# Giving a query with an empty bucket all keys alike, in a bucketed attention kernel

## The chip, the cores and the metric

One core of one Trainium2 chip runs the whole program in one launch. The metric is device time in microseconds from start to end of an execution; the median of several runs is given. TensorE (PE) multiplies matrices, VectorE (DVE) reduces and combines, ScalarE (ACT) does exponentials and copies, GpSimd (POOL) does elementwise work in SBUF, SyncE (SP) issues the DMAs.

## The reference

Attention with hashed buckets over 2 batches, 8 heads, 768 positions of 64 values, and behind it two feed-forward stages. Only the attention is touched:

```python
q_bits = (np.einsum('bhsd,dk->bhsk', q, proj) > 0)      # six bits a query
k_bits = (np.einsum('bhsd,dk->bhsk', k, proj) > 0)
mask = q_bucket[..., :, None] == k_bucket[..., None, :]
scores = scale * np.matmul(q, k.transpose(0, 1, 3, 2))
scores = np.where(mask, scores, -1000000000.0)
scores = scores - np.max(scores, axis=-1, keepdims=True)
attn = np.exp(scores)
attn = attn / (np.sum(attn, axis=-1, keepdims=True) + 1e-09)
out = np.matmul(attn, v)
```

A query whose bucket holds no key ("lone") has -1e9 in its whole row; after the subtraction of the maximum every entry is 0, so it takes all 768 keys with equal weight. The stages behind are max(x w1, x w2, x w3) w_out on 1536 tokens, and a gated one with 2048 hidden columns.

## The kernel before, in words

The order of each engine's work is written out by hand, one function for each engine, and semaphores order the engines among each other. The attention has 96 tiles, each of 128 queries against 768 keys. They are taken in 32 groups of three; n is the group, p = n // 4 the pair of heads and st = n % 4 the stage in the pair.

For tile i: TensorE (`scores`, L1027) multiplies the queries by the keys twice, the second time (76 rows) adding 2^100 for each bit that differs, so the mask is part of the product, with its sign turned. VectorE (`row_max`, L790) takes the minimum of the negated scores into one column of `neg_max`. ScalarE (`exp_tile`, L624) writes `probs[i % 6]` and adds up the row into `sums`. VectorE (`invert_sums`, L795) adds 1e-9 and takes the reciprocal, and GpSimd (`norm`, L468) multiplies the tile by it. TensorE (`turn_probs`, L1047) transposes the tile in two halves into one of three banks of a ring (`psR`), ScalarE and VectorE copy these to `probs_t` (L637, L810), and TensorE (`times_values`, L1054) multiplies by the values.

What waits for what around the change: `scores(i)` waits for the exponential of tile i - 2 (L1031), since there are two score banks. `turn_probs` waits for the norm of its tile and for a free bank. Within group n VectorE's order is row_max(3n), copy_turned, invert_sums(3n-1, 1) (one tile), row_max(3n+1), invert_sums(3n, 2) (two tiles), in stage 2 make_bits, in even groups x_lo_unit, row_max(3n+2), copy_turned (L845 to L863). GpSimd's order is norm(3n-1), norm(3n), norm(3n+1), then in stages 0 and 1 make_qk_hi and make_qk_lo (L447 to L458) for the next pair, in stage 2 mark (L460), and in stages 2 and 3 of pairs 4 to 6 three steps of sums_of_x (L506), in the last pair first_block (L531 to L548). ScalarE also copies the turned q and k of the next pair (L621), and TensorE needs the same ring banks for them. SyncE moves the split q and k and the marks to their places by DMA once GpSimd has made them (L340 to L360), and loads ahead.

For a lone query of the kernel before, the exponentials are those of the keys with the fewest differing bits, since each differing bit adds 2^100 and the minimum is subtracted.

The program's second part, the two feed-forward stages, follows from about 232 us on and is not edited. GpSimd splits the weights there (L445, L490, L579), VectorE has instructions with two SBUF inputs there (`h_lo`, L937, for one).

Of the kernel before, what the change touches and what calls it, by code (L numbers as in the profile page):

```python
# [5 lines left out]
def lsh_attention_ffn(nc, q, k, v, proj, w1, w2, w3, w_out, w_in2, w_out2, out):  # L6
    F32, F32R, BF16 = mybir.dt.float32, mybir.dt.float32r, mybir.dt.bfloat16
    I32 = mybir.dt.int32
    ALU, ACT, AX = mybir.AluOpType, mybir.ActivationFunctionType, mybir.AxisListType
    ts = bass.ts  # L10

    B, H, S, D = q.shape
# [3 lines left out]
    P = 128  # L16
# [8 lines left out]
    UPS2 = F2 // P  # L25
    NEG_SCALE = -1.0 / 8.0
    assert D == 64 and H * D == DM and NBITS == 6
    MASKED = 2.0 ** 100
    CONSTS = 2
    WARM_UP = 22  # L30

# [3 lines left out]
    PROBS = 6  # L35
# [44 lines left out]
    with ctx:  # L80
        def sb(name, shape, dt):
            return ctx.enter_context(nc.sbuf_tensor(name, shape, dt))

        def sem(name):
            return ctx.enter_context(nc.semaphore(name))
# [12 lines left out]
        neg_max = sb("neg_max", [P, 6], F32)  # L98
        sums = sb("sums", [P, 6], F32)
        guarded = sb("guarded", [P, 6], F32)  # L100
        inv = sb("inv", [P, 6], F32)
        with ExitStack() as attention:
            probs = [attention.enter_context(nc.sbuf_tensor(f"probs{i}", [P, S], F32)) for i in range(PROBS)]

# [105 lines left out]
        scores_ready = sem("scores_ready")  # L210
        max_ready = sem("max_ready")
        probs_ready = sem("probs_ready")
        sums_guarded = sem("sums_guarded")
        inv_ready = sem("inv_ready")
        probs_normed = sem("probs_normed")
# [218 lines left out]
        def _(pool):  # L434
# [32 lines left out]

            def norm(i):  # L468
                pool.wait_ge(inv_ready, 2 * (i // 3) + (2 if i % 3 == 2 else 1))
                pool.tensor_scalar(probs[i % PROBS][:, :], probs[i % PROBS][:, :], inv[:, i % 6:i % 6 + 1], 1.0,  # L470
                                   ALU.mult, ALU.mult).then_inc(probs_normed, 1)

            def raw_part(k, name):

# [56 lines left out]
            for n in range(GROUPS + 1):  # L531
                p, st = n // 4, n % 4
                if n > 0:
                    norm(3 * n - 1)
                if n < GROUPS:
                    norm(3 * n)
                    norm(3 * n + 1)
                    if st == 2 and p + 1 < PAIRS:
                        mark(p + 1)
                    if st < 2 and p + 1 < PAIRS:  # L540
                        make_qk_hi(2 * p + 2 + st)
                        make_qk_lo(2 * p + 2 + st)
                    if PAIRS // 2 <= p < PAIRS - 1 and st >= 2:
                        for step in range(6 * (p - PAIRS // 2) + 3 * st - 6, 6 * (p - PAIRS // 2) + 3 * st - 3):
                            if step < 16:
                                sums_of_x(step)
                    if p == PAIRS - 1:
                        first_block(st)  # L548
# [232 lines left out]
        def _(dve):  # L781
# [13 lines left out]
            def invert_sums(i, count):  # L795
                cols = slice(i % 6, i % 6 + count)
                turn = 2 * (i // 3) + (1 if i % 3 == 2 else 0)
                dve.wait_ge(probs_ready, i + count)
                dve.tensor_scalar(guarded[:, cols], sums[:, cols], 1e-9, None, ALU.add).then_inc(sums_guarded, 1)
                dve.wait_ge(sums_guarded, turn + 1)  # L800
                if i >= 6:
                    dve.wait_ge(probs_normed, i - 6 + count)
                dve.reciprocal(inv[:, cols], guarded[:, cols]).then_inc(inv_ready, 1)  # L803

            def copy_turned(i, j):
# [20 lines left out]
            dve.tensor_scalar(marks[:, 3:4], row[:, :], float(3 * NBITS), None, ALU.is_ge).then_inc(marks_made, 1)  # L826
            dve.tensor_scalar(marks[:, 1:2], row[:, :], float(MARKS), MASKED, ALU.is_ge, ALU.mult).then_inc(marks_made, 1)
            dve.wait_ge(marks_made, 3)
# [16 lines left out]
            for n in range(GROUPS + 1):  # L845
                p, st = n // 4, n % 4
                if n < GROUPS:
                    row_max(3 * n)
                if n > 0:
                    copy_turned(3 * n - 3, 0)  # L850
                    invert_sums(3 * n - 1, 1)
                if n < GROUPS:
                    row_max(3 * n + 1)
                if n < GROUPS:
                    invert_sums(3 * n, 2)
                    if st == 2 and p + 1 < PAIRS:
                        make_bits(("bits", p + 1), slice(0, P))
                if n >= 4 and n % 2 == 0:
                    x_lo_unit(n // 2 - 2)
                if n < GROUPS:  # L860
                    row_max(3 * n + 2)
                if n > 0:
                    copy_turned(3 * n - 1, 1)  # L863
# [383 lines left out]
```

## Time and profile before

| what | value |
|---|---|
| median of 3 runs | 693.0 us (692.21 to 694.57) |
| the profiled execution's own time | 692.77 us |
| its span (first to last instruction) | 690.3 us |
| PE busy | 679.4 us, 98% |
| DVE busy | 378.3 us, 55%, 683 instructions |
| ACT busy | 274.7 us, 40% |
| POOL busy | 395.0 us, 57% |
| granted TensorE clock | full throughout |

The shares are over the whole span. A busy VectorE or GpSimd costs time only where TensorE, or the last chain of waits, stands behind it. So each row below is read with its place in time: the loop over groups lasts from about 14 to 232 us.

### The profile page before, as it was taken

Reading aid. Unit: us, or ns where it says so; the run is one execution under the profiler, and the core shown is the slowest. Engines: PE = TensorE matmul, PEld = TensorE weight load, DVE = VectorE, ACT = ScalarE, POOL = GpSimd, SP = SyncE. Lnnn points to the kernel's source line nnn. Section 1 sums busy time; section 2 is a strip of 40 time slices with the busy share of each in tenths; the row PEclk is TensorE's granted clock in tenths of the full one; section 3 lists DMA queues with packets and bytes.
Section 4 is the critical chain, followed back from the end, with each engine's and each line's share of the span. In section 5 each row is a group of like instructions: output and inputs, shape, how many; then the busy total and the mean of one; then the engine's idle time right before and its main releaser. Section 6 shows DMA issues by size and latency. Waiting matters only on the chain.

```text
span 690.3 us, 11104 instructions
## 1 busy us (share of the span) xinstructions
PE 679.4 (98%) x3970; PEld 592.9 (86%) x3970; DVE 378.3 (55%) x683; ACT 274.7 (40%) x582; POOL 395.0 (57%) x448
## 2 busy tenths in 40 slices
PE   7899999999999999999999999999999999999998
PEld 5677777777777699999999999999999999999996
DVE  5767676767677799879688613222222242222222
ACT  3877787877777530110105113222222232222222
POOL 4755755688876899778843123444444444444441
PEclk9999999999999999999999999999999999999999
DMA  5845736628342111101010111222222152222202
GB/s 116 201 108 131 174 85 148 162 81 185 97 110 85 32 31 30 31 32 54 24 46 1 62 31 46 62 62 62 61 62 62 46 168 65 71 64 64 71 20 91
DMA packets 67141, 54.07 MB, mean 78 GB/s; under 512 B 29200, under 2 KB 56080, under 8 KB 67088
## 3 DMA queue, kind: packets, MB, share of 16 engines
q1 hardware_dynamic: 66768, 53.36, 29.1%
q8 instruction: 32, 0.52, 0.3%
q14 instruction: 21, 0.17, 0.1%
q10 hardware_dynamic: 320, 0.01, 0.0%
HBM read 32.51 MB, written 3.15 MB: 52 GB/s over the span
## 4 chain that ended last, share of the span: by engine, by line
PE 91%; DVE 5%; DMA 1%; SPq 1%; issue 1%; ACT 0%; DVEq 0%; ACTq 0%
PE psS L1043 10%; PE psO L1065 9%; PE psR L1051 9%; PE psR L1113 8%; PE psR L1111 8%; PE psR L1112 8%; PE psS L1111 5%; PE psS L1113 5%; PE psS L1112 5%; PE psS L1213 4%; PE psS L1214 4%; PE psS L1212 4%; DVE probs L869 2%; PE psR L1012 2%; PE psO L1214 1%; PE psO L1213 1%
## 5 line engine op out<-in xcount | busy, mean ns | idle before, releaser
L445 POOL TENSOR_SCALAR w_hi<-w_raw 128x512 fp32r<-128x512 f32 (+2 forms) x134 | 84.1, 629 | 199.8 <-PE psO L1214 129.7
L979 DVE TENSOR_TENSOR probs_t<-psR,probs_t 128x384 f32<-128x384 f32 x64 | 35.7, 557 | 181.9 <-ACT probs_t L761 181.9
L470 POOL TENSOR_SCALAR probs<-probs,inv 128x768 f32<-128x768 f32 x96 | 86.1, 905 | 66.4 <-DVE inv L803 65.3
L761 ACT ACTIVATE probs_t<-psR 128x384 f32<-128x384 f32 x64 | 31.5, 492 | 188.0 <-PE psR L1113 188.0
L792 DVE TENSOR_REDUCE neg_max<-psS 128x1 f32<-128x768 f32 x96 | 91.7, 956 | 20.3 <-PE psS L1043 15.9
L579 POOL TENSOR_TENSOR w_lo<-w_raw,w_hi 128x512 fp32r<-128x512 f32 (+1 forms) x68 | 90.6, 1332 | 5.7
L628 ACT ACTIVATE probs<-psS,neg_max 128x768 f32<-128x768 f32 x96 | 86.4, 900 | 11.8 <-DVE neg_max L792 11.8
L1051 PE MATMUL psR<-ident,probs 128*128 128x128 f32 x576 | 74.6, 273 | 1.5 <-ACT w_raw L621 0.9
L637 ACT ACTIVATE probs_t<-psR 128x384 f32<-128x384 f32 x128 | 59.4, 491 | 34.2 <-PE psR L1051 34.1
L1051 PEld LDWEIGHTS psR<-ident,probs 128*128 128x128 f32 x576 | 66.5, 141 | 6.0 <-POOL probs L470 1.9
L1065 PE MATMUL psO<-probs_t,v_raw 128*64 128x384 f32 x384 | 68.8, 494 | 0.0
L1111 PE MATMUL psR<-x_hi,w_hi 128*128 128x384 f32 x176 | 59.1, 336 | 0.0
L1113 PE MATMUL psR<-x_hi,w_lo 128*128 128x384 f32 x176 | 59.0, 335 | 0.0
L1112 PE MATMUL psR<-x_lo,w_hi 128*128 128x384 f32 x176 | 58.9, 335 | 0.0
L1065 PEld LDWEIGHTS psO<-probs_t,v_raw 128*64 128x64 f32 x384 | 24.8, 136 | 30.9 <-issue 30.7
L1214 PE MATMUL psS<-w_hi,stacks 128*128 128x512 f32 x128 | 50.4, 394 | 0.0
L1213 PE MATMUL psS<-w_lo,stacks 128*128 128x512 f32 x128 | 50.4, 393 | 0.0
L1212 PE MATMUL psS<-w_hi,stacks 128*128 128x512 f32 x128 | 49.8, 389 | 0.0
L490 POOL TENSOR_TENSOR w_lo<-w_raw,w_hi 128x256 fp32r<-128x256 f32 x52 | 45.2, 876 | 0.3
L982 DVE TENSOR_TENSOR stacks<-probs_t,stacks 128x384 fp32r<-128x384 f32 x64 | 37.5, 587 | 3.8
L1113 PE MATMUL psR<-h_hi,w_lo 128*128 128x384 f32 x116 | 39.0, 336 | 0.0
L1111 PE MATMUL psR<-h_hi,w_hi 128*128 128x384 f32 x116 | 38.9, 336 | 0.0
(204 smaller groups left out, 1533.8 us busy)
## 6 DMA issues: line engine op xcount, KB each, us to landing
w_raw<-in_moe_w_in SPq DMA_DIRECT2D x32, 256.0 KB, 2.6
w_raw<-in_moe_w_out SPq DMA_DIRECT2D x32, 256.0 KB, 2.7
w_raw<-in_moe_w SPq DMA_DIRECT2D x9, 512.0 KB, 3.8
h_lo<-w_hi SPq DMA_DIRECT2D x22, 192.0 KB, 3.6
h_hi<-w_hi SPq DMA_DIRECT2D x18, 192.0 KB, 3.7
w_raw<-in_q SPq DMA_DIRECT2D x16, 192.0 KB, 3.3
w_raw<-in_k SPq DMA_DIRECT2D x16, 192.0 KB, 4.1
v_raw<-in_v SPq DMA_DIRECT2D x16, 192.0 KB, 2.6
```

The lines of the kernel that those rows point to most:

```text
L445: return pool.tensor_scalar(dst, src, 1.0, 1.0, ALU.mult, ALU.mult)
L470: pool.tensor_scalar(probs[i % PROBS][:, :], probs[i % PROBS][:, :], inv[:, i % 6:i % 6 + 1], 1.0, ALU.mult, ALU.mult).then_inc(probs_norm ...
L579: pool.tensor_tensor(w_lo[:, cols], src, f32(w_hi[:, cols]), ALU.subtract).then_inc(done, 1)
L628: act.activation(probs[i % PROBS][:, :].rearrange("p (a b) -> p a b", a=2), psS[i % 2][:, :, 0:HALF], ACT.Exp, bias=neg_max[:, i % 6:i % 6 ...
L792: dve.tensor_reduce(neg_max[:, i % 6:i % 6 + 1], psS[i % 2][:, :, 0:HALF], AX.XY, ALU.min).then_inc(max_ready, 1)
L1051: mm = pe.transpose(o[:, ts(c, P)], probs[i % PROBS][:, ts(j * TH + c, P)], ident[:, :])
L1065: mm = pe.matmul(psO[a * D:(a + 1) * D, 0:HALF], v_raw[p % 2][a][:, c, :], probs_t[u % 2][:, a, c, :], start=c == 0, stop=c == NT - 1)
L1111: pe.matmul(o, wh, xh, start=c == 0, stop=False)
L1112: pe.matmul(o, wh, xl, start=False, stop=False)
L1113: mm = pe.matmul(o, wl, xh, start=False, stop=c == len(terms) - 1)
L1213: pe.matmul(acc[t], g_part(g % 2, 0)[:, ts(t, P)], wl, start=False, stop=False)
L1214: mm = pe.matmul(acc[t], g_part(g % 2, 1)[:, ts(t, P)], wh, start=False, stop=f == UPS2 - 1)
```

## The change

`invert_sums` first derives two values from the row maximum: `lone` is 2^60 where the minimum of the negated scores is at least 2^99 (no key in the bucket) and 0 elsewhere, `lone_sums` is 768 times that. The sum's addition of 1e-9 also adds `lone_sums`, now a tensor in SBUF, and `norm` adds `lone` to each entry before it multiplies by the reciprocal. The wait for the norms of six tiles ago moves from before the reciprocal to the front of the function.

```diff
+    LONE = 2.0 ** 60
...
+        lone = sb("lone", [P, 6], F32)
+        lone_sums = sb("lone_sums", [P, 6], F32)
...
             def norm(i):
                 pool.wait_ge(inv_ready, 2 * (i // 3) + (2 if i % 3 == 2 else 1))
-                pool.tensor_scalar(probs[i % PROBS][:, :], probs[i % PROBS][:, :], inv[:, i % 6:i % 6 + 1], 1.0,
-                                   ALU.mult, ALU.mult).then_inc(probs_normed, 1)
+                pool.tensor_scalar(probs[i % PROBS][:, :], probs[i % PROBS][:, :], lone[:, i % 6:i % 6 + 1],
+                                   inv[:, i % 6:i % 6 + 1], ALU.add, ALU.mult).then_inc(probs_normed, 1)
...
             def invert_sums(i, count):
                 cols = slice(i % 6, i % 6 + count)
                 turn = 2 * (i // 3) + (1 if i % 3 == 2 else 0)
-                dve.wait_ge(probs_ready, i + count)
-                dve.tensor_scalar(guarded[:, cols], sums[:, cols], 1e-9, None, ALU.add).then_inc(sums_guarded, 1)
-                dve.wait_ge(sums_guarded, turn + 1)
                 if i >= 6:
                     dve.wait_ge(probs_normed, i - 6 + count)
+                dve.wait_ge(max_ready, i + count)
+                dve.tensor_scalar(lone[:, cols], neg_max[:, cols], MASKED / 2, LONE, ALU.is_ge, ALU.mult).then_inc(lone_found, 1)
+                dve.tensor_scalar(lone_sums[:, cols], neg_max[:, cols], MASKED / 2, S * LONE, ALU.is_ge,
+                                  ALU.mult).then_inc(lone_found, 1)
+                dve.wait_ge(probs_ready, i + count)
+                dve.wait_ge(lone_found, 2 * turn + 2)
+                dve.scalar_tensor_tensor(guarded[:, cols], sums[:, cols], 1e-9, lone_sums[:, cols], ALU.add,
+                                         ALU.add).then_inc(sums_guarded, 1)
+                dve.wait_ge(sums_guarded, turn + 1)
                 dve.reciprocal(inv[:, cols], guarded[:, cols]).then_inc(inv_ready, 1)
```

## Rows read from the trace of the kernel before

**Rows 1.** Busy time by stretch: busy us (instructions) of each engine, clock, DMA share.

```profile
70.00:97.50 27.50, 27.50 (x192) 20.25 (x188) 19.27 (x39) 21.16 (x47) 16.58 (x17) 1.00 0.59 136
```

**Rows 2.** Waits from 30 to 232 us: total us, times, longest.

```profile
DVE guarded L799 <- ACT probs L628: 31.8, 30, 1.1
...
DVE neg_max L792 <- PE psS L1043: 15.1, 22, 1.2
```

**Rows 3.** Timeline, stage 0's end and stage 1: start, duration us, instruction, [idle before].

```profile
153.30 1.05 ACT L621 ACTIVATE w_raw<-psR,qk_scale 128x384 f32<-128x384 f32 x2
...
154.12 1.15 PE L1051 MATMUL psR<-ident,probs 128*128 128x128 f32 x9
...
155.81 1.15 PE L1051 MATMUL psR<-ident,probs 128*128 128x128 f32 x9
...
157.35 0.14 DVE L799 TENSOR_SCALAR guarded<-sums 128x1 f32<-128x1 f32 x1
157.53 0.16 DVE L803 RECIPROCAL inv<-guarded 128x1 f32<-128x1 f32 x1
...
157.69 0.96 DVE L792 TENSOR_REDUCE neg_max<-psS 128x1 f32<-128x768 f32 x1
...
159.71 0.17 DVE L799 TENSOR_SCALAR guarded<-sums 128x2 f32<-128x2 f32 x1 [1.06 <-ACT probs L628]
...
161.99 0.42 PE L1043 MATMUL psS<-h_lo 128*128 128x384 f32 x1
```

**Rows 4.** Timeline at the start: two independent 128x1 instructions of VectorE.

```profile
2.23 0.14 DVE L826 TENSOR_SCALAR marks<-row 128x1 f32<-128x1 int32 x1
2.29 0.14 DVE L827 TENSOR_SCALAR marks<-row 128x1 f32<-128x1 int32 x1
```

**Rows 5.** Timelines: VectorE's instructions that fell on running ones of GpSimd.

```profile
24.06 0.90 POOL L470 TENSOR_SCALAR probs<-probs,inv 128x768 f32<-128x768 f32 x1
...
24.73 0.26 DVE L799 TENSOR_SCALAR guarded<-sums 128x2 f32<-128x2 f32 x1 [1.06 <-ACT probs L628]
...
377.38 2.02 POOL L579 TENSOR_TENSOR w_lo<-w_raw,w_hi 128x768 fp32r<-128x768 f32 x1
...
377.62 2.20 DVE L937 TENSOR_TENSOR h_lo<-probs_t,h_lo 128x384 fp32r<-128x384 f32 x1
```

**Rows 6.** GpSimd: the norm's form (busy us, mean ns), then two instructions of the timeline.

```profile
L470 POOL TENSOR_SCALAR probs<-probs,inv 128x768 f32<-128x768 f32 x96 | 86.1, 905 | 66.4 <-DVE inv L803 65.3
...
154.97 0.83 POOL L445 TENSOR_SCALAR w_hi<-w_raw 128x768 fp32r<-128x768 f32 x1
...
155.89 1.82 POOL L458 TENSOR_TENSOR w_lo<-w_raw,w_hi 128x768 fp32r<-128x768 f32 x1
```

**Rows 7.** Timeline of a stage 2 group, after one addition of a stage 3.

```profile
150.79 1.00 POOL L519 TENSOR_TENSOR early<-early 128x384 f32<-128x384 f32 x1
...
162.85 1.82 POOL L458 TENSOR_TENSOR w_lo<-w_raw,w_hi 128x768 fp32r<-128x768 f32 x1
...
164.31 0.14 DVE L799 TENSOR_SCALAR guarded<-sums 128x1 f32<-128x1 f32 x1
...
167.55 0.62 DVE L787 TENSOR_SCALAR bits<-psR,marks 128x384 f32<-128x384 f32 x1 [0.51 <-PE psR L1023]
...
168.55 0.94 DVE L792 TENSOR_REDUCE neg_max<-psS 128x1 f32<-128x768 f32 x1
...
169.53 0.91 ACT L628 ACTIVATE probs<-psS,neg_max 128x768 f32<-128x768 f32 x1
...
170.81 0.94 PE L1043 MATMUL psS<-stacks 128*128 128x384 f32 x4
```

**Rows 8.** The chain of waits at the start: start us, us, what.

```profile
28.73 0.97 DVE neg_max L792
...
31.78 0.52 PE psR L1051 x3
```

**Rows 9.** Timeline at the start: GpSimd beside that one-tile call.

```profile
27.96 1.83 POOL L458 TENSOR_TENSOR w_lo<-w_raw,w_hi 128x768 fp32r<-128x768 f32 x1
```

More of the change, by code:

```diff
@@ L212, in lsh_attention_ffn @@
         probs_ready = sem("probs_ready")
+        lone_found = sem("lone_found")
         sums_guarded = sem("sums_guarded")
```

## The prediction

> **What bounds the kernel now.** I read the stretches of time first. In the attention loop (about 20 to 232 us) TensorE is busy for the whole of each stretch, 27.50 of 27.50 us in the one shown [rows 1], at full granted clock, while VectorE has 19.3 and GpSimd 16.6 us of work. So a change on VectorE and GpSimd costs nothing until it makes TensorE wait. Behind the loop nothing is edited; what the loop loses, the program loses.
>
> The waits of the loop come second [rows 2]. VectorE waits 31.8 us for the exponentials (30 times, 1.06 us each), and 15.1 us for TensorE's scores. That is where added VectorE work may disappear.
>
> Third, the timeline of one group of three tiles [rows 3]. In stages 0 and 1 of a pair a group lasts 6.96 us. VectorE calls invert_sums twice: for one tile (guarded 157.35, reciprocal 157.53, next row maximum 157.69: nothing waits there, so it is work in line), and for two tiles (guarded 159.71, after the 1.06 us wait).
>
> **The change part by part.** 64 calls get two flag instructions each, 128 in all; 64 guarded additions get a second tensor; 96 norms get a second per-partition scalar and an addition. No DMA is added or moved; the kernel's stores and loads keep their places, except that they may start later where GpSimd is late.
>
> 1. *Flags.* Two independent 128x1 instructions start 0.065 us apart [rows 4]. The tile's guarded addition now waits for the second flag, one dependent step of 0.18 us (157.35 to 157.53, [rows 3]). In the one-tile call: 0.065 + 0.18 = 0.25 us, plus 0.02 for the wider addition (my value; from 0 to 0.06 by the spread of small instructions). So the next row maximum, its exponential, and the two norms behind it come 0.27 us later. In the two-tile call the flags need only the maximum that has just been taken, and lie in the 1.06 us wait. The earlier wait for probs_normed asks for norms of two groups ago: nothing. Behind the waiting flag stand the guarded addition, reciprocal and row maximum. 0.27 us by itself is hidden: scores of tile 3n+3 need exponential 3n+1 and come 2.2 us after it (161.99 against 159.71, where that exponential ends the wait, [rows 3]), and VectorE waits for scores before row maximum 3n+2.
>
> 2. *The second tensor of the guarded addition.* This is what I expect to cost. The addition now has two inputs in SBUF. The trace before has no small one beside a busy GpSimd, but it has large ones: an L937 of 384 elements issued at 377.62 took 2.20 us, where GpSimd's instruction ran from 377.38 to 379.40; it ended 0.42 us (384 elements) after that one. And the one 128x2 guarded addition that fell on a running norm (24.06 to 24.96) took 0.26 instead of 0.17 us and ended at 24.99 [rows 5]. So VectorE is held until GpSimd's instruction ends. Bounds: 0 to the whole rest of GpSimd's instruction (1.8 us); I take the rest plus 0.03.
> The Trainium skill (SBUF — State Buffer, Who interferes with whom) says that a VectorE instruction with two SBUF inputs, or in a two-port mode, is fully blocked by a GpSimd instruction that reads SBUF and was issued first; the rows are of that kind, though none has one element.
>
> 3. *The norm.* It takes 0.905 us with one pointer [rows 6]; the same shape with two constants takes 0.83. A second pointer thus costs 0 to 0.07; I take the middle, 0.035. That the addition in place of a multiplication changes the loop is bounded by the two-tensor instruction, 1.82 us for 768 elements [rows 6], so up to +0.92. I take none: the norm already does two operations in one pass.
> The Trainium skill (GPSIMD Engine Reference, 3.1) has loop bodies of up to two operations bound by the port at 1.03 cycles an element; by that the norm stays at 0.9 us, but no run yet shows another pair of operations.
>
> Now the steps in a pair of heads, with D the lateness of row maximum 3n+1. Stage 0: D = 0.27. GpSimd's two norms, qk_hi and qk_lo follow back to back, so qk_lo (155.89 to 157.71, [rows 6]) ends at 157.71 + 0.27 + 0.02 + 0.07 = 158.07. Stage 1: the one-tile addition would start at 157.60, so it is held until 158.10, and the reciprocal comes at 158.12 instead of 157.53: D = 0.59. Stage 2: qk_lo (162.85 + 1.82 = 164.67) now ends at 165.35, the reciprocal comes at 165.40, where without change it is 164.31 + 0.18 = 164.49: D = 0.9 [rows 7]. That goes through the exponential into the two-tile reciprocal, and so bits starts at about 167.88 instead of 167.55, row maximum 3n+2 at 168.88 instead of 168.55, its exponential at 169.86 instead of 169.53, and it ends (1.02 us) at 170.88. TensorE starts the scores that need it at 170.81, with its weights 0.03 earlier: a stall of 0.15 us counting the signal. Stage 3 has no GpSimd work beside the one-tile call in pairs 0 to 3, and D falls back to 0.27. Four pairs like this: 0.6 us.
>
> In pairs 4 to 6 GpSimd also runs three additions of 1.0 us in stages 2 and 3, up to the next one-tile call (150.79, [rows 7]). GpSimd being 0.7 to 1.0 late, the addition falls on them: D = about 0.9 in stages 3 and 0. In stage 0 ACT's two copies of q and k (153.30, 1.05 us long) come 0.9 later, and the transposes from 154.12 on reuse their banks; the slack there is about 0.5 us (154.12 + 0.33 for one half, against 153.82): a stall of 0.4. Four such places and the stage 2 ones: I put 1.8 us on pairs 4 to 6.
>
> At the start the pipeline is empty and the chain of waits runs through VectorE: row maximum at 28.73, exponential, reciprocal, bits, TensorE at 31.78 [rows 8]. The one-tile addition before it would start at 28.63, while GpSimd's instruction runs from 27.96 to 29.79 [rows 9]; held until 29.82 and 0.1 for GpSimd's own lateness, it puts 1.4 us on the chain, and 0.1 for two transposes. The last group, with nothing behind to hide in: 0.3.
>
> Sum: 1.5 + 0.6 + 1.8 + 0.3 = 4.2 us, on the profiled execution's own 692.77 (its span 690.3 and 2.5 around it): 697.0. The median of the runs is 0.2 higher; I leave the forecast at 697.0. With no cost of the pointer the stage 2 stalls go and 2.7 remains (695.5); with 0.07 all are longer, 5.3 (698.1). The likeliest case's own range is 695.2 to 699.
>
> **Rivals.**
> - *No hold (ends on the other side, no slower).* If an addition of one or two elements slips in beside GpSimd, only the 0.27 us of each one-tile call remains. At the start it is on the chain (0.3), elsewhere hidden by 2.2 us of slack; 0.1 to 0.5 for the rest: +0.4 to +0.8, 693.4. For it: 128x1 additions with one input took 0.14 us with GpSimd running (164.31, [rows 7]). Against: [rows 5]. It decides at the first such addition: below about 0.3 us of hold a call, TensorE never waits.
> - *GpSimd becomes the bound.* If the add and multiply pair runs in a slower loop, the two norms of a call end late for the transposes, which start at 155.81 [rows 3] and read the second of them after two halves (0.66 us), while it ends at 154.97: slack 1.5. At 1.2 us a norm (+0.3) that holds, but the holds of step 2 grow with each norm in front of them, about 0.5 us a group over 31 groups: +16, 709. At the two-tensor price GpSimd has 3 x 1.82 + 0.9 + 1.9 = 8.3 us in stages 0 and 1 against the group's 6.96, and with the holds I put 1.5 on each of the 31: +47, 740. For it: nothing in the trace shows any pair but multiply, multiply on GpSimd. Against: such a pass runs at 1.1 ns an element, hardly more than reading them.
> - *Faster.* Only by a shift that lets collisions of GpSimd and VectorE behind the loop (L937's 2.20 us) fall more kindly, a few tenths: 692.5.
>
> **How the numbers follow.** Forecast, held addition: 0.55. No hold: 0.24. GpSimd bound: 0.17. Faster: 0.04. A difference under 0.3% (2.1 us) can't be told from none. The held case is slower by more than that except at its lowest end (0.53 of 0.55), with GpSimd bound 0.16: slower 0.69. No hold and the low end: same 0.27. Faster 0.04. The range runs from 693.0, which leaves out the faster case and a bit of the no-hold one, to 706, which takes in norms up to 1.05 us (+0.15, about +10) and leaves out about 0.14.
>
> **What would show it.** Held: L799's one-tile durations (0.14 now) rise to 0.4 to 0.6 us in stages 1 and 2 and to 1.2 at the start, two-tile ones stay near 0.2; TensorE shows idle gaps of 0.1 to 0.5 us before scores and transposes; VectorE's flags start 0.065 us apart. Norm mean 0.94 us. The loop is 4 us longer, what is behind it unchanged. I am wrong if one-tile additions stay at 0.16 us, if the norm's mean is over 1.0 us, or if the time is lost behind 232 us.

## The result, and the profile after

| | before | changed |
|---|---|---|
| median | 692.84 us (8 runs, 691.93 to 694.57) | 696.77 us (8 runs, 695.01 to 697.62) |
| ratio | | 1.0053, 95% interval 1.0039 to 1.0067 |
| profiled execution | 692.77 us, span 690.3 | 696.38 us, span 694.6 |
| DVE, POOL busy | 378.3, 395.0 us | 401.3, 404.6 us |

The forecast was 697.0 us. The added time lies mostly where the prediction put it, at the start and in pairs 4 to 6. The start of the profiled execution lost twice what was forecast, and the part that was not forecast is only in part explained (below).

Where it is lost is seen from the start of each group's multiplication by the values (`times_values`), changed minus before, in us, worked out from the two timelines:

```
group         3     7     11    15    19    20    23    24    27    28    31
shift       3.02  3.04  3.05  3.08  3.10  3.40  3.79  4.08  4.46  4.76  4.78
```

So 3.0 us are lost before group 3, 0.1 in pairs 1 to 3, 1.7 in pairs 4 to 6 (groups 19 to 28), 0.1 at the end. Behind the loop 0.5 us come back: the span is 4.3 longer. In 11 of the 12 other kernels below 0.5 to 0.7 us come back as well (in the one with a single changed instruction nothing does), so this is most likely a slow spot of the one profiled execution of before.

The shift before group 3 compares two single executions, and it differs by itself from one to the next. The kernels below with the longer norm alone, the flags alone and the scalar form have medians like before, and yet shifts of 1.1, 1.6 and 1.7 us at group 4. In the scalar form's profile 0.9 us of it is one wait of TensorE for a DMA, which is short in the profile of before (first row: scalar form, second: before):

```profile
21.10 0.62 PE L1059 MATMUL psS<-h_lo,h_hi 76*128 76x384 f32 x2 [1.15 <-DMA h_lo<-w_hi]
...
19.96 0.62 PE L1043 MATMUL psS<-h_lo,h_hi 76*128 76x384 f32 x2 [0.28 <-DMA h_lo<-w_hi]
```

**The hold.** The timeline of the changed kernel at the start, GpSimd's qk_lo and VectorE's one-tile call (start, us, engine, instruction, [idle before]); it answers to [rows 8, 9]:

```profile
28.20 1.83 POOL L464 TENSOR_TENSOR w_lo<-w_raw,w_hi 128x768 fp32r<-128x768 f32 x1
28.38 0.14 DVE L807 TENSOR_SCALAR lone<-neg_max 128x1 f32<-128x1 f32 x1
28.44 0.15 DVE L808 TENSOR_SCALAR lone_sums<-neg_max 128x1 f32<-128x1 f32 x1
...
28.69 1.36 DVE L812 SCALAR_TENSOR_TENSOR guarded<-sums,lone_sums 128x1 f32<-128x1 f32 x1
...
30.16 0.94 DVE L798 TENSOR_REDUCE neg_max<-psS 128x1 f32<-128x768 f32 x1
...
31.39 0.55 PE L1063 MATMUL psR<-ident,probs 128*128 128x128 f32 x3 [0.68 <-POOL probs L476]
...
33.18 0.55 PE L1063 MATMUL psR<-ident,probs 128*128 128x128 f32 x3 [1.25 <-DVE bits L793]
```

One element in each partition takes 1.36 us, and ends at 30.05, 0.02 after GpSimd's instruction (30.03). The row maximum behind it comes at 30.16 instead of 28.73, and the last transposes of the group at 33.18 instead of 31.78: 1.4 us.

In stages 1 and 2 of pair 5 the same is seen, to answer to [rows 3, 6, 7]:

```profile
160.05 1.84 POOL L464 TENSOR_TENSOR w_lo<-w_raw,w_hi 128x768 fp32r<-128x768 f32 x1
...
161.06 0.83 DVE L812 SCALAR_TENSOR_TENSOR guarded<-sums,lone_sums 128x1 f32<-128x1 f32 x1
...
167.31 1.82 POOL L464 TENSOR_TENSOR w_lo<-w_raw,w_hi 128x768 fp32r<-128x768 f32 x1
...
168.03 1.13 DVE L812 SCALAR_TENSOR_TENSOR guarded<-sums,lone_sums 128x1 f32<-128x1 f32 x1
```

They end at 161.89 and 169.16, within 0.03 us of GpSimd's ends (161.89, 169.13). The second hold is 0.30 us longer: GpSimd's instruction comes 7.26 us after the one before it, VectorE's 6.97 us, since the first hold made GpSimd late.

The same holds for all traces of this case together, counted over instructions of VectorE that started while one of GpSimd's had over 0.3 us left to run. Of 117 one-element additions with two tensors, 116 were held and ended 0.00 to 0.02 us after GpSimd's; the other one had started in the same 10 ns as it. All 39 two-element ones were held. Of 368 one-element instructions with one tensor and constants none was. An addition that starts ahead of GpSimd's instruction is not held either: in the changed kernel's group 1 it comes at 22.12, GpSimd's at 22.24, and it takes 0.16 us.

**The norm**, from the page's groups (busy us, mean ns), to answer to [rows 6]:

```profile
L476 POOL TENSOR_SCALAR probs<-probs,lone,inv 128x768 f32<-128x768 f32 x96 | 94.1, 987 | 63.6 <-DVE inv L815 63.6
```

A second pointer and an addition cost 0.08 us, just over the upper end of the bound for the pointer; there is no slower loop.

**The clock**, by stretches of the changed kernel (us; busy PE, PEld, DVE, ACT, POOL; granted clock; DMA share, GB/s):

```profile
32.00:33.00 1.00, 0.00 (x0) 0.00 (x0) 0.81 (x4) 0.89 (x4) 0.38 (x1) 1.00 1.06 234
33.00:34.00 1.00, 0.82 (x5) 0.85 (x6) 1.00 (x3) 0.07 (x1) 1.00 (x2) 0.77 1.05 206
34.00:35.00 1.00, 1.00 (x5) 0.90 (x4) 0.36 (x1) 0.93 (x2) 1.00 (x2) 0.50 1.05 234
35.00:36.00 1.00, 1.00 (x7) 1.00 (x6) 0.95 (x2) 0.00 (x0) 0.13 (x1) 0.50 0.27 64
36.00:37.00 1.00, 1.00 (x6) 1.00 (x5) 0.86 (x6) 0.67 (x2) 0.00 (x0) 0.52 0.14 35
37.00:38.00 1.00, 1.00 (x6) 0.58 (x7) 0.31 (x2) 1.00 (x3) 0.85 (x1) 1.00 0.08 18
```

TensorE had been idle for 0.68 and then 1.25 us; behind that its granted clock is 0.50 (1.2 GHz) for 3.4 us. The shift grows there from 1.4 to 3.0 us: 1.6 us, more than the stall itself. Whether the idle time brought the fall is taken up at the end of the experiments.

**Pairs 4 to 6.** TensorE's weight loads that waited for another engine between 150 and 182 us (pairs 4 and 5):

```profile
152.85 0.31 PEld L1063 LDWEIGHTS psR<-ident,probs 128*128 128x128 f32 x3 [0.31 <-POOL probs L476]
174.57 0.65 PEld L1055 LDWEIGHTS psS<-stacks 128*128 128x128 f32 x4 [0.19 <-ACT probs L634]
180.94 0.31 PEld L1063 LDWEIGHTS psR<-ident,probs 128*128 128x128 f32 x3 [0.29 <-POOL probs L476]
```

In stage 2 it waits for the exponential of tile 3n+2, behind stage 3 for the second norm of a call. What delays that norm is seen in the stage 3 call of pair 5: VectorE's additions and even its flags run into GpSimd's work.

```profile
175.29 1.01 POOL L525 TENSOR_TENSOR early<-early,x_lo 128x384 f32<-128x384 f32 x1
...
175.51 0.80 DVE L812 SCALAR_TENSOR_TENSOR guarded<-sums,lone_sums 128x1 f32<-128x1 f32 x1
...
177.35 0.98 POOL L476 TENSOR_SCALAR probs<-probs,lone,inv 128x768 f32<-128x768 f32 x1
...
177.55 0.81 DVE L808 TENSOR_SCALAR lone_sums<-neg_max 128x2 f32<-128x2 f32 x1
```

### The profile page after: what moved, and what is told of

Its sections match the earlier page's. It is cut to its first block, busy times and chain, and to the rows that moved or that the text cites. A ratio compares the mean times of both kernels' runs of the same rounds, so it can differ in the third digit from the quotient of the medians.

```text
span 694.6 us, 11296 instructions
## 1 busy us (share of the span) xinstructions
PE 682.7 (98%) x3970; PEld 594.7 (86%) x3970; DVE 401.3 (58%) x811; ACT 274.1 (39%) x582; POOL 404.6 (58%) x448
## 4 chain that ended last, share of the span: by engine, by line
PE 89%; DVE 5%; issue 2%; DMA 1%; POOL 1%; ACT 1%; SPq 0%; DVEq 0%; ACTq 0%; POOLq 0%
PE psR L1123 9%; PE psR L1125 9%; PE psR L1124 9%; PE psO L1077 8%; PE psS L1055 8%; PE psR L1063 7%; PE psS L1123 6%; PE psS L1124 6%; PE psS L1125 6%; PE psS L1225 4%; PE psS L1226 4%; PE psS L1224 4%; DVE neg_max L798 2%; PE psR L1024 2%; DVE guarded L812 1%
## 5 line engine op out<-in xcount | busy, mean ns | idle before, releaser
L476 POOL TENSOR_SCALAR probs<-probs,lone,inv 128x768 f32<-128x768 f32 x96 | 94.1, 987 | 63.6 <-DVE inv L815 63.6
L1063 PE MATMUL psR<-ident,probs 128*128 128x128 f32 x576 | 76.6, 276 | 3.2 <-DVE bits L793 1.2
```

The costliest lines, as they stand in the source:

```text
L1063: mm = pe.transpose(o[:, ts(c, P)], probs[i % PROBS][:, ts(j * TH + c, P)], ident[:, :])
```

## The experiments

Theory A: a guarded addition with a second SBUF tensor is held until GpSimd's running instruction ends. Rival B: the added instructions in line and the longer norms cost the time. Rival C: the fall of the clock has another cause than TensorE's idle time. Rival D: the longer norm alone overfills GpSimd in pairs 4 to 6. Ratios are to the kernel before on the same chip, where 693.17, 692.72 and 693.45 us were its medians in the three sets of runs.

**The second tensor alone** (kernel before, `zeros` is a tensor set once):

```diff
-dve.tensor_scalar(guarded[:, cols], sums[:, cols], 1e-9, None, ALU.add)
+dve.scalar_tensor_tensor(guarded[:, cols], sums[:, cols], 1e-9, zeros[:, cols], ALU.add, ALU.add)
```

> The kernel before, whose guarded addition gets a tensor of zeros as second input in all 64 calls; no flags, norm as before. Theory A (the addition is held until GpSimd's running instruction ends): the one-tile addition at 28.38 us, under GpSimd's 27.96 to 29.79, takes about 1.4 us; TensorE then idles over 1 us at 32, its clock falls for about 2.5 us as in the changed kernel, together +2.7 to +3.0 at the start; later holds of 0.2 to 0.5 us in stages 1 and 2 stay hidden in pairs 1 to 3 and cost 0.3 to 0.8 in pairs 4 to 6. +3.0 to +3.8 us. Rival B (the extra instructions and the longer norm do it): L799's one-tile duration stays at 0.16, no change, under +0.3 us.

Measured 694.55 us, ratio 1.0020 (1.0010 to 1.0031). The addition is held:

```profile
28.77 1.83 POOL L460 TENSOR_TENSOR w_lo<-w_raw,w_hi 128x768 fp32r<-128x768 f32 x1
...
29.20 1.41 DVE L801 SCALAR_TENSOR_TENSOR guarded<-sums,zeros 128x1 f32<-128x1 f32 x1
```

B is out for this part. The expected sum of 3.0 to 3.8 us was too high: TensorE idles 1.33 us behind the hold, but in this execution the clock stayed at 1.00, and from group 19 to 31 the shift grows by 0.3 us, as fast as from group 3 to 19. Without the longer norm the loop absorbs the holds.

**The longer norm alone** (a column of zeros as addend):

```diff
-pool.tensor_scalar(probs, probs, inv[:, c:c + 1], 1.0, ALU.mult, ALU.mult)
+pool.tensor_scalar(probs, probs, zeros[:, c:c + 1], inv[:, c:c + 1], ALU.add, ALU.mult)
```

> The kernel before, whose norm adds a column of zeros and multiplies by the reciprocal; no flags, guarded addition as before. Theory A: the norm takes 0.987 us as in the changed kernel, but the pair of norms is read 1.0 to 1.5 us after it ends, so only the start feels it: +0.3 to +0.6 us. Rival B (96 x 0.08 = 7.9 us of GpSimd time shows in part): +2 to +4 us.

Measured 693.58 us, ratio 1.0004 (0.9995 to 1.0012). The 7.6 us of added GpSimd work are hidden.

**The flags alone** (the changed kernel with the addition and the norm of before):

> The changed kernel with the guarded addition and the norm of the kernel before: the two flags a call and their waits remain, 128 instructions, but nothing uses what they find. Theory A: row maximum 3n+1 comes 0.26 to 0.31 us later in each group and TensorE doesn't notice except at the start: +0.2 to +0.5 us. Rival B (each of the 31 delays shows): +5 to +9 us.

Measured 692.89 us, ratio 0.9996 (0.9986 to 1.0007). 128 instructions cost nothing that can be measured. Flags and norms by themselves cost nothing, so B is out as it stands; that the longer norm adds to the cost of the holds is shown further down.

**The share as a per-partition scalar** in one-tile calls, all results as in the changed kernel:

```diff
+if count == 1:
+    dve.tensor_scalar(guarded[:, cols], sums[:, cols], lone_sums[:, cols], 1e-9, ALU.add, ALU.add)
+else:
     dve.scalar_tensor_tensor(guarded[:, cols], sums[:, cols], 1e-9, lone_sums[:, cols], ALU.add, ALU.add)
```

> The changed kernel, in whose one-tile calls the share comes as a per-partition scalar (one tensor input) and not as a second tensor; all results the same. Theory A with a scalar not using the shared port: the one-tile additions take 0.16 us everywhere, no gap at 32 us, clock stays full: +0.7 to +1.1 over the kernel before, 3 us under the changed one. Theory A with a scalar using it: durations and time as in the changed kernel, +3.9. Rival B (length of the line and the norm): +3.5 to +4, with additions of 0.16 us.

Measured 693.36 us, ratio 0.9996 (0.9987 to 1.0005). The 32 scalar forms (count x, min/median/max ns) and one of them beside a running GpSimd:

```profile
L813 DVE TENSOR_SCALAR guarded<-sums,lone_sums x32: 214/214/216, 23.4 to 231.7; 128x1 f32<-128x1 f32 x32
...
29.02 1.83 POOL L464 TENSOR_TENSOR w_lo<-w_raw,w_hi 128x768 fp32r<-128x768 f32 x1
29.69 0.21 DVE L813 TENSOR_SCALAR guarded<-sums,lone_sums 128x1 f32<-128x1 f32 x1
```

The scalar costs 0.05 us more than the second tensor where that is not held (0.16 us). It is never held: in the five kernels that use it, none of the 48 that started beside a GpSimd instruction with over 0.3 us to run. The whole loss goes, with flags and longer norms in place.

**The scalar in group 2's one-tile call only** (`if i == 5`):

> The changed kernel, whose one-tile addition of group 2 alone takes the share as a per-partition scalar; all other calls keep the second tensor. Theory A (about 3.0 us are lost in group 2, by the hold and by the slower clock behind it, 1.7 us in pairs 4 to 6): the gap at 32 us and the clock's fall go, shifts of the later groups stay; 1.5 to 2.2 us over the kernel before, 1.5 to 2.5 under the changed one. Rival B (the loss is spread over all groups): within 0.5 us of the changed kernel.

Measured 695.68 us, ratio 1.0040 (1.0023 to 1.0057), about 1 us under the changed kernel's ratio of 1.0053, with intervals that overlap, and so less of a gain than the expected 1.5 to 2.5. The gap of 1.25 us and the fall behind it are gone, but in this execution the clock fell earlier, between 20.4 and 23.8 us, and the shift grew by 1.1 us there:

```profile
20.00:26.00 6.00, 5.49 (x28) 4.86 (x26) 3.33 (x11) 4.00 (x9) 4.78 (x5) 0.72 0.90 232
```

The shifts are 1.9 us at group 7 and go to 3.8 at group 28: pairs 4 to 6 lose their 1.8 us unchanged.

**One instruction of 64** (kernel before, second tensor only at `i == 5`):

> The kernel before, where one instruction of 64 is changed: the one-tile addition of group 2 takes a tensor of zeros as second input. Theory A: held about 1.4 us under GpSimd's qk_lo, on the chain of the start: +1.2 to +1.6 us with full clock, up to +3 in executions whose clock falls behind the gap. Rival B (a single hold of a 1-element addition can't cost more than GpSimd's remaining 1.8 us, and TensorE has slack by then): under +0.3 us.

Measured 695.24 us, ratio 1.0030 (1.0019 to 1.0042): about 2.1 us by the ratio from one addition of one element, which took 1.33 us. In the profile the hold adds 1.1 us to TensorE's idle time; where the rest is lost is not shown. Half of the 6 executions had a clock under 0.999, and they were no slower than the others (both halves have medians of 695.2 to 695.3). In the profiled one the clock fell between 17.6 and 21.0 us, ahead of the hold, and not behind it.

**The scalar in pairs 4 to 7 only** (`if count == 1 and i >= 53`):

> The changed kernel with the share as a per-partition scalar in the one-tile calls from group 18 on (pairs 4 to 7); the calls before keep the second tensor. Theory A (pairs 4 to 6 lose 1.7 us by the hold): shifts stay at the start's level of about 3.0 us from group 3 to the end, 1.2 to 1.8 us under the changed kernel, 695.2. Rival D (the longer norm alone overfills GpSimd in pairs 4 to 6): the shifts of groups 20 to 28 stay, under 0.5 us gained.

Measured 695.02 us, ratio 1.0032 (1.0020 to 1.0045). The shift is 4.49 us at group 4, 4.54 at group 20 and 4.57 at group 28 (in this execution the clock fell twice at the start, at 21.3 and at 34.9 us). Pairs 4 to 6 lose nothing without the hold, D is out.

**The norm of before, holds kept** (the addend is left out):

> The changed kernel with the norm of the kernel before (one pointer, no addend; the addend for lone queries is left out). Flags and second tensors stay. Theory A (the norms' 0.08 us each lengthen the holds, since GpSimd's next instructions come later): norm 0.905 us, holds in stages 1 and 2 shorter by 0.1 to 0.4 us; the start still loses 1.3 to 3 us, pairs 4 to 6 at most 1.2 instead of 1.7: 0.4 to 1.3 us under the changed kernel. Rival B (the longer norm is most of the cost): 3 us under it.

Measured 695.57 us, ratio 1.0044 (1.0030 to 1.0059). The shift is 3.04 us at group 20 and 3.16 at group 28. So pairs 4 to 6 lose their 1.7 us only where hold and longer norm come together; either alone is absorbed.

This start loses 3.0 us too, and at full clock throughout: here the holds fall on both groups, 1.59 us in group 1 and 1.01 in group 2, and TensorE idles 2.44 and 1.33 us behind them (0.94 and 0.50 before).

```profile
27.24 0.99 PE L1063 MATMUL psR<-ident,probs 128*128 128x128 f32 x6 [2.44 <-ACT w_raw L627]
...
34.77 0.52 PE L1063 MATMUL psR<-ident,probs 128*128 128x128 f32 x3 [1.33 <-DVE bits L793]
...
28.00:30.00 2.00, 2.00 (x18) 1.97 (x16) 1.58 (x3) 1.57 (x4) 1.92 (x4) 1.00 1.16 214
36.00:38.00 2.00, 2.00 (x17) 1.57 (x17) 1.84 (x7) 1.83 (x6) 0.56 (x1) 1.00 0.02 3
```

**Small matmuls into the idle time**, to keep the clock:

```diff
+if n == 2 and (i, j) == (3 * n - 1, 1):
+    keep_running(18)
 turn_probs(i, j)
```

> The changed kernel with 18 small matmuls into the unused psO bank queued on TensorE in group 2, ahead of the transpose that waits for the bits bank. All holds stay. Theory A (the idle gap of 1.25 us lowers the granted clock to 0.5 for about 2.7 us, which costs 1.4 to 1.8 us): clock 1.00 throughout, the gap's own time stays, 1.3 to 1.8 us under the changed kernel, 695.2. Rival C (the fall of the clock is no consequence of the gap, and comes from something else in that stretch): clock and time as in the changed kernel, or 0.3 us longer by the added matmuls.

> The changed kernel with 24 small matmuls ahead of the waiting transposes of group 1 and 18 ahead of those of group 2. Theory A: the granted clock stays 1.00 in nearly all executions, the idle time itself stays: 694.9 to 695.5, like the executions of the changed kernel with full clock (695.0). Rival C (the clock's fall has another cause): clock under 0.999 in half of the executions or more, as in the run with the fill in group 2 alone, and 695.4 or more.

Measured 695.43 us, ratio 1.0037 (1.0021 to 1.0053), with the fill in group 2, and 696.50, ratio 1.0044 (1.0032 to 1.0057), with both. Neither settles it. The profile of the first shows why: in this execution the hold fell on group 1, where it had no fill, and the clock fell behind it.

```profile
22.67 1.82 POOL L464 TENSOR_TENSOR w_lo<-w_raw,w_hi 128x768 fp32r<-128x768 f32 x1
22.75 1.75 DVE L812 SCALAR_TENSOR_TENSOR guarded<-sums,lone_sums 128x1 f32<-128x1 f32 x1
...
27.20 0.99 PE L1063 MATMUL psR<-ident,probs 128*128 128x128 f32 x6 [2.42 <-ACT w_raw L627]
...
30.00:32.00 2.00, 2.00 (x9) 1.78 (x7) 1.81 (x6) 1.59 (x4) 1.74 (x1) 0.51 0.83 161
```

Which group of the start is hit hangs on 0.1 us: here qk_lo starts 0.08 us ahead of the addition, in the changed kernel's profile 0.12 us behind it. With both fills 4 of 5 executions kept the clock, but three of these took 696.5 to 696.8 us, near the changed kernel's 696.77; the fills' own cost wasn't measured apart. In the profiled one the clock fell between 20.3 and 23.7 us, ahead of both fills.

**Scalar form and one-tile call moved** behind row maximum 3n+1:

> The changed kernel with the share as a per-partition scalar in one-tile calls, and the one-tile call moved behind row maximum 3n+1, into the wait for the exponential; all results the same. Theory A (what is left of the cost is the one-tile call's 0.6 us in line, which moves to where VectorE waits): the start loses nothing, 0.2 to 0.7 us under the run with the scalar alone, at or slightly under the kernel before, 692.7. Rival B (norm 3n-1 comes 1 us later and makes GpSimd late for the transposes): +0.5 to +3 us.

Measured 693.50 us, ratio 1.0005 (0.9993 to 1.0016): no gain over the unmoved one. The moved norm 3n-1 now runs beside the two-tile addition, which still has two tensors, and that one is held (median 676 ns instead of 164).

**Scalar form with fills of 12 and 8** small matmuls:

> The changed kernel with the share as a per-partition scalar in all one-tile calls, and 12 and 8 small matmuls ahead of the waiting transposes of groups 1 and 2; all results the same. Theory A (a third of the executions even of the kernel before have a clock under 0.999, by the gaps at the start): clock full in all, at or up to 0.5 us under the run with the scalar alone, 692.6 to 693.2. Rival C: no change against it, 693.4, with a spread as wide.

Measured 692.73 us, ratio 0.9994 (0.9983 to 1.0004), in a set where the kernel before had 693.45. No difference that can be told; 5 of 11 executions still had a clock under 0.999, where all were expected to have the full clock; it was 1 of 11 without the fills and 7 of 16 for the kernel before in the same set. Like the scalar form alone it gives the changed kernel's results at the time of before.

**What the traces say of the clock.** Behind an idle time of 1.25 us in group 2 it fell in two profiles (the changed kernel's and that of the scalar in pairs 4 to 7). Behind idle times of 1.33 and 1.34 us at the same place it stayed full in three (second tensor alone, norm of before, one instruction of 64). Behind 2.42 us in group 1 it fell, behind 2.44 us it did not. And in five profiles it fell ahead of any hold, at 12.8, 17.6, 20.4, 20.3 and 21.3 us (flags alone, one instruction of 64, scalar in group 2 only, both fills, scalar in pairs 4 to 7), though TensorE's idle times ahead of the last three (0.97 us at most) were no longer than those of the kernel before (up to 1.07 us), whose clock stayed full. So an idle time of this length neither suffices for a fall nor is it needed; what decides is open.

## Why the prediction was right

- *Added work in line, 0.27 us a one-tile call, hidden but at the start*: right in the medians; the kernel with the flags alone is as fast as before.
- *The hold until GpSimd's end, plus 0.03*: right in kind and size. It was taken from an instruction of 384 elements and holds for one element: the ends agree within 0.03 us at the start and in stages 1 and 2. Its second row, the 128x2 addition of 0.26 us, has one tensor and so was no case of the two-tensor kind; such instructions are held too, but not always (see the end).
- *The second pointer 0.035 us, no slower loop*: the loop was right, the pointer cost 0.08. By the prediction's own working that would have made 5.3 us and 698.1 (with 0.07), 1.3 us above the measured time; the terms of this sum, and of the 2.7 us without a pointer cost, are not given.
- *Stage 2 stalls, 0.15 us a pair, 0.6 in all*: too high. Pairs 1 to 3 lose 0.1 together, though the norm is longer than taken; pair 0 lies in the start.
- *Pairs 4 to 6, 1.8 us*: 1.7 measured, partly in another place. The stage 2 exponential was named. The banks of the q and k copies in stage 0 were not what TensorE waited for; it was the second norm of the stage 3 call, 0.3 us late. (The slack given as about 0.5 us there comes to 0.63 by its own two times, 154.45 and 153.82.) The prediction had the two-tile flags as free in the 1.06 us wait; there they are held too, up to 0.8 us, and push the reciprocal.
- *The start, 1.5 us*: the stall is 1.4. The step had no term for the granted clock, 1.6 us more in the profiled execution. Over the executions: one of 8 of the changed kernel had a mean clock of 0.999 or more, and took 695.0 us; the other 7 have a median of 696.9. Of the kernel before, 51 of 75 had it (692.7), 24 had not (693.8); with the scalar form, 10 of 11. So with the holds in place falls are more frequent and go with longer times, but the traces above do not show that the gap brings the fall, and the fills, which were to show it, did not. By the ratios, which stand over many executions, the start costs about 2.1 us (one instruction of 64) to 2.2 (scalar in pairs 4 to 7), 0.6 to 0.7 more than forecast.
- *The last group, 0.3 us*: 0.1.

The mechanism was right, and the nearness of the number is in part luck: in the profiled executions 1.6 us of clock were missing, 0.5 were too much in stage 2, 0.2 too much at the end and 0.1 each at the start and in pairs 4 to 6, and 0.5 us came back behind the loop. By the ratios the start (about 2.1 us) and pairs 4 to 6 (1.5 us, from 1.0053 against 1.0032; 1.7 in the profile) make up the measured 3.7 us.

## What to carry to other kernels

Count the SBUF tensors that a small VectorE instruction reads while GpSimd works: in all traces here the second one made it wait until GpSimd's running instruction had ended (1.36 us for one element), and a per-partition scalar did not (0.21 us). A hold in the steady loop may be free, and the same hold in the filling of the pipeline cost about its full length or more: 2.1 us for one of 1.33. Price added work on two engines together: in pairs 4 to 6 the holds on VectorE alone and the longer norms on GpSimd alone are absorbed, and both together cost 1.7 us. And compare the start of two single profiles with care: here kernels of the same median differ by over 1 us in it.

## What the runs showed that was not expected

- A per-partition scalar from SBUF costs VectorE 0.05 us (214 ns against 160) and isn't held by GpSimd.
- VectorE's 128x2 instructions with one SBUF tensor can be held as well (lone_sums 0.81 us under a norm), its 128x1 ones never (0.14 us beside GpSimd's qk_lo). Over all traces 49 of 76 such 128x2 ones were held, and the other 27 had all started within 0.12 us of GpSimd's instruction, as `lone` did 0.08 us ahead of that lone_sums (177.47, 0.17 us).
- At the start an order that differs by 0.1 us decides which group is hit by a hold.
